# Twenty-four transposes of the identity on TensorE ahead of the first projections

## The reference, cut to what matters

```python
# q, k, v: (2, 8, 768, 64), proj: (64, 6)
q_bits = (q @ proj > 0);  k_bits = (k @ proj > 0)
bucket = sum(bits * 2 ** arange(6))                  # for q and for k
scores = 0.125 * q @ k.T, and -1e9 where the buckets of q and k differ
attn   = exp(scores - max) / (sum + 1e-9)
x = (attn @ v), heads side by side                   # (2, 768, 512)
u = x + real(fft(fft(x, axis=1), axis=2))
x2 = u + relu(layernorm(u) @ w_ch1) @ w_ch2
out = (sigmoid(causal_conv5(x2)) * (x2 @ w_val)) @ w_out
```

## Time and profile before

| | |
|---|---|
| median of 3 runs | 647.86 us (647.46 to 648.29) |
| the profiled execution, its own time | 647.66 us |
| its span, first to last instruction | 646.0 us |
| TensorE busy | 618.5 us, 96% of the span |
| VectorE / ScalarE / GpSimd busy | 353.4 / 316.9 / 245.6 us |
| mean granted TensorE clock recorded | 0.997 |

### The profile page before, as it was taken

How to read it: one execution, slowest core, us unless ns; L and a number is a source line. 1 busy time by engine, 2 the same in 40 slices (tenths; PEclk the granted TensorE clock), 3 DMA queues, 4 the chain that set the end, 5 groups by cost and what they waited for, 6 DMA issues and landing times.

```text
span 646.0 us, 11034 instructions
## 1 busy us (share of the span) xinstructions
PE 618.5 (96%) x3730; PEld 502.5 (78%) x3730; DVE 353.4 (55%) x587; ACT 316.9 (49%) x608; POOL 245.6 (38%) x199
## 2 busy tenths in 40 slices
PE   2999999999999999887999999999999999999998
PEld 1767777767767766886888888888888888888786
DVE  2888888888888885986211111115533333439820
ACT  2777777777787763465222222225332333354242
POOL 6533443334334342844322333325544444303140
PEclk9999999999999999999999999999999999999999
DMA  5662323323332000100222111431322212000202
GB/s 130 201 142 64 86 62 85 85 74 103 91 85 61 14 13 1 49 2 2 66 65 63 53 49 62 166 95 33 97 56 59 55 59 65 16 2 1 82 17 97
DMA packets 34265, 42.12 MB, mean 65 GB/s; under 512 B 3520, under 2 KB 22208, under 8 KB 34240
## 3 DMA queue, kind: packets, MB, share of 16 engines
q1 hardware_dynamic: 32512, 37.77, 20.4%
q0 software_dynamic: 1728, 4.02, 2.5%
HBM read 38.63 MB, written 3.15 MB: 65 GB/s over the span
## 4 chain that ended last, share of the span: by engine, by line
PE 86%; DVE 7%; issue 2%; POOL 2%; ACT 2%; DMA 1%; SPq 0%; ACTq 0%; DVEq 0%; POOLq 0%
PE banks L1487 21%; PE banks L1475 20%; PE banks L1285 12%; PE banks L1302 10%; PE banks L1349 9%; PE banks L1582 4%; PE banks L1241 2%; PE banks L1566 2%; PE banks L1422 2%; DVE x_then_u_then_gate L1160 1%; PE banks L1325 1%; PE banks L1247 1%; PE banks L1357 1%; POOL row_sums_and_differences L526 1%; PE banks L1396 1%
## 5 line engine op out<-in xcount | busy, mean ns | idle before, releaser
L1147 DVE SCALAR_TENSOR_TENSOR h_lo<-banks,h_hi 128x512 fp32r<-128x512 f32 x64 | 35.3, 557 | 181.3 <-ACT h_hi L809 181.3
L954 DVE TENSOR_REDUCE row_min<-banks 128x1 f32<-128x768 f32 x96 | 91.8, 956 | 33.0 <-PE banks L1285 32.5
L663 ACT ACTIVATE prob<-banks,row_min 128x768 f32<-128x768 f32 x96 | 87.0, 906 | 35.7 <-DVE row_min L954 35.6
L1475 PE MATMUL banks<-unT_hi,w_hi 128*128 128x512 f32 (+1 forms) x256 | 86.5, 338 | 0.2 <-DVE h_lo L1147 0.2
L1475 PE MATMUL banks<-unT_hi,w_lo 128*128 128x512 f32 (+1 forms) x256 | 86.2, 337 | 0.0
L1475 PE MATMUL banks<-unT_lo,w_hi 128*128 128x512 f32 (+1 forms) x256 | 86.2, 337 | 0.0
L1349 PE MATMUL banks<-ident,prob 128*128 128x128 f32 x576 | 79.3, 273 | 2.4 <-ACT probT L342 1.3
L549 POOL TENSOR_TENSOR w_lo<-w_stage,w_hi 128x512 fp32r<-128x512 f32 x32 | 45.3, 1416 | 80.9 <-ACT w_hi L726 80.9
L1349 PEld LDWEIGHTS banks<-ident,prob 128*128 128x128 f32 x576 | 68.4, 140 | 7.7 <-issue 2.4
L554 POOL TENSOR_TENSOR w_lo<-w_stage,w_hi 128x512 fp32r<-128x512 f32 x32 | 42.2, 1318 | 74.9 <-ACT w_hi L731 74.9
L1302 PE MATMUL banks<-probT,v_in 128*64 128x384 f32 x384 | 69.0, 494 | 0.7 <-DVE probT L342 0.7
(11 more groups left out here) (147 smaller groups left out, 1188.2 us busy)
## 6 DMA issues: line engine op xcount, KB each, us to landing
w_stage<-in_moe_w_ch SPq DMA_DIRECT2D x64, 256.0 KB, 2.8
q_raw<-in_q SPq DMA_DIRECT2D x32, 192.0 KB, 3.2
k_raw<-in_k SPq DMA_DIRECT2D x32, 192.0 KB, 3.6
v_in<-in_v SPq DMA_DIRECT2D x16, 192.0 KB, 2.8
out<-y_out SPq DMA_DIRECT2D x12, 256.0 KB, 2.0
seq_tables_sb<-in_dft POOLq DMA_DIRECT2D x6, 386.0 KB, 3.6
wvo_stage<-in_moe_w_val SPq DMA_DIRECT2D x1, 1024.0 KB, 5.8
wvo_stage<-in_moe_w_out SPq DMA_DIRECT2D x1, 1024.0 KB, 8.9
```

The lines of the kernel that those rows point to most:

```text
L663: act.activation(prob[s % 2][:, :, :], s_tile(s), ACT.Exp, bias=row_min[:, s:s + 1], scale=-1.0, accum_out=row_sum[:, s:s + 1]).then_inc(e ...
L954: dve.tensor_reduce(row_min[:, s:s + 1], s_tile(s), AX.XY, ALU.min).then_inc(min_ready, 1)
L1147: dve.scalar_tensor_tensor(out=h_lo[:, slot, at:at + size], in0=h_bank[c], scalar=0.0, in1=h_hi[:, slot, at:at + size].bitcast(F32), op0=A ...
L1475: op = pe.matmul(h_bank[c], w_[:, slot, kb, :], x_[:, kb, at:at + size], start=(kb == 0 and m == 0), stop=(kb == KB - 1 and m == 2))
```

## The change

Behind the wait for the identity and before the wait for `w_ready`, TensorE transposes the identity 24 times into the same 128 columns of bank 7. Nobody reads the result, no semaphore is raised, and nothing is removed or moved.

```diff
@@ -383,6 +383,8 @@
         LAG = 3
+
+        WARM = 24
@@ -1366,6 +1368,8 @@
             pe.wait_ge(consts_ready, 7)
 
+            for n in range(WARM):
+                pe.transpose(PS[:, 7, 0:P], ident[:, :], ident[:, :])
             pe.wait_ge(w_ready, 2)
             pe.wait_ge(codes_loaded, 16)
```

## The result

| | kernel before | changed kernel |
|---|---|---|
| median | 647.68 us (20 runs, 646.79 to 648.44) | 646.86 us (20 runs, 645.13 to 647.84) |
| ratio | | 0.9984, 95% interval 0.9978 to 0.9990 |
| profiled execution | 647.66 us, span 646.0 us | 646.16 us, span 644.5 us |
| mean recorded clock of it | 0.997 | 0.992 |

The kernel became 0.8 us faster, 0.16%, where 1.0 us was forecast.

The account below looks back on a forecast made before the run. TensorE, busy 96% of the span, was taken as the bound, at a low unrecorded clock until about 20.3 us. Free transposes and a faster prologue gave 647.66 - 0.95 = 646.7 us, range 644.6 to 648.1 us.

Parts of the forecast that it names:

- The cost: At the start, 24 transposes at 0.215 us each end inside the wait for `proj` and `w_k`; taken as 0.
- The rise: During or just behind the starting transposes, TensorE's clock goes to the high level, between 6.6 and 9.2 us.
- the 0.68 us of L1241: Prologue's eight L1241 matmuls, 1.54 us on the chain, take about 0.85 us at the high clock; 0.68 us saved.
- the 0.28 us of L1247: Prologue's first L1247 shrinks from 0.70 to 0.42 us at the high clock; 0.28 us saved.
- The fall: Between the transposes and the first scores TensorE is about 30% busy, so the clock falls about when the scores start.
- the comparison of three stretches: Busy shares ahead of a possible fall: 62% near 280 us held, 47% before 303.7 us fell, about 30% to come.
- the 62% stretch: From 280.30 to 284.90 us, TensorE busy 2.87 of 4.60 us, thinnest found at the high level without a fall.
- a long low stretch: From the first scores, clock low 5.9 us as before, only 0.95 us earlier: 646.7 us, likeliest case, chance 0.38.
- The short rival: From the first scores, clock low only 3.4 us, as at 303.7 us: 1.9 us saved, 645.8 us, chance 0.21.
- the row minimum of slot 2: VectorE's step that started at 20.40 us before; its new start was said to give the whole gain.
- No fall: Clock stays high through the first scores: 0.95 + 0.64 + 1.2 = 2.8 us saved, 644.8 us, chance 0.23.
- The low stretch near 303 us: Late in the kernel, said to move the end up to about 1.2 us either way, unrelated to the transposes.

Follow-up runs that it names:

- c3: The changed kernel with nothing altered, profiled once more (third look): 646.88 us, one run.
- c2: The changed kernel with nothing altered, profiled once more (second look): 647.01 us, one run.
- e7: 48 transposes at the start instead of the changed kernel's 24: 648.38 us, ratio 1.0004 to the kernel before.
- e4: The changed kernel plus 7, 7 and 8 transposes in the layer norm gaps near 300 us: 645.97 us, ratio 0.9978 to the kernel before.
- e1: The changed kernel plus 18 transposes in the gap ahead of the first scores: 644.76 us, ratio 0.9956 to the kernel before.
- e6: The changed kernel with 12 plain float32 matmuls of the identity in place of the 24 transposes: 646.66 us, ratio 0.9983 to the kernel before.
- c1: The changed kernel with nothing altered, profiled once more (first look): 646.57 us, one run.
- e5: The changed kernel plus 5 and 18 transposes before the first scores, 12 near 280 us, and 7, 7, 8 near 300 us: 644.05 us, ratio 0.9942.
- e8: The kernel before plus only late transposes, 12 near 280 us and 7, 7, 8 near 300 us: 646.78 us, ratio 0.9984.
- e2: The kernel before plus only 10 transposes in the gap ahead of the first scores, none at the start: 646.04 us, ratio 0.9975.

## Why the prediction was right

**The cost.** Taken at 0 with 0.2 to 0.4 us to spare, it was 0 with 0.4 to 1.9 us to spare (idle time ahead of L1243 in c3 and c2). L1243 starts at 8.94 instead of 8.83 us because `w_k` came later, 8.88 instead of 8.73 us, behind a load of `proj` that took 3.97 instead of 3.86 us. That all write the same columns did not matter: they followed each other at 0.21 us and less, not 0.40. Where they do outlast the cover, as the 48 of e7, the real work comes later by the excess, 2.3 us.

**The rise.** Forecast between 6.6 and 9.2 us, it came at 6.4 us in the profile, near 8.8 in e7, and in c3 (5.38 us for 24) not before the last transpose, yet L1243 was fast in every profile with 24. So the 0.68 us of L1241 and the 0.28 us of L1247 were nearly got: 1.54 to 0.90 us and 0.70 to 0.46 us, 0.88 us together. With L1243 starting 0.11 us later the first scores came 0.78 us earlier than before, at 13.66 and not at 13.49 us. Transposes alone raised the clock, as the earlier trace rows had shown once. The rule of the Trainium skill, page "TensorE: Matmul & The Clock Gate", section "Part 4: PE-mode transpose", that they do not count as busy, does not hold here: the clock rose while TensorE had done nothing but transposes, and 24 transposes and 12 matmuls of the same length acted alike.

**The fall.** The step on which the most hung was the comparison of three stretches: 62% busy, held; 47%, fell; about 30% to come. The coming one was 26% (1.47 of 5.60 us) in the profile, and the clock fell in all five profiles. With the gap filled it stayed. So the fall was rightly forecast.

The comparison behind it is weaker than it looked. The fall of e4 came behind 5.60 us that were 70% busy and that of c3 behind 5.60 us that were 65% busy (3.63 us, 6.40 to 12.00), both thicker than the 62% stretch that had held. And that 62% stretch, with its gap of 1.7 us, did not always hold either: of the eleven profiles in which it is unfilled, the clock fell within 1.7 us of the gap's end in four (e1, e4, e6, c1, at 282.6 to 284.0 us). A busy share read off one profile does not settle whether the clock falls, and that the three stretches of the comparison came out in order was in part luck.

The longest single gap ahead of the first scores was 2.50 us. The Trainium skill, same page, section "HAM oscillation — how this bites in real kernels", ties a fall to idle gaps longer than this one; three falls, this one, that of e4, and the one near 300 us behind gaps of 1.14 us at most, came without such a gap. The trace of before also held a second fall, which the prediction did not count: at 645.0 us, 2.1 us behind the last matmul, where TensorE has no work left.

**What the fall leaves.** Forecast 0.95 us with a long low stretch and 1.9 us with a short one. Measured at 248 us: 0.92, 0.82 and 0.42 with a long one, 1.50 and 1.36 with a short one. The long one was the likeliest case and its gain is that of the median. It was not the case of the profiled execution, and the median is one of a mix: two profiles of five had the short stretch, and the twenty runs of the changed kernel lie between 2.5 us below and 0.2 us above the median of before, late low stretches included. The long stretch was also longer than forecast (6.8 us, not 5.9) and began 1 to 3 us before the first scores, not with them. The short rival was sized 0.4 to 0.5 us too high: I took the row minimum of slot 2 as the end of the gain. It started 1.8 us earlier in the profile, at 17.66 + 0.96 = 18.6 us instead of 20.40, but slot 3's scores then waited 0.55 us for ScalarE and came 1.45 us earlier. So that moment does not give the whole gain, as the prediction said it would; slot 3's scores do.

**No fall.** Forecast 2.8 us, of which 1.2 us, and not TensorE's own 1.9, for the part in which the exponential leads. e1 measured 2.70 us at 247 us. This sum was made for the rival and holds for the kernel with its gap filled.

**What I treated as outside.** The low stretch near 303 us was called worth up to 1.2 us either way and left out of the sum. That was fair for this change and missed how much it carries of the run-to-run spread. These are medians of runs sorted by their mean recorded clock, those of before from e1's comparison and those of the changed kernel from the result. In that mean 3.4 us at the low level are worth 1.7 / 646 = 0.0026:

| recorded clock | low stretches of 3.4 us | before (26 runs) | changed (20 runs) |
|---|---|---|---|
| 0.999 to 1.000 | none, or less than one | 646.82 us, 7 runs | |
| 0.997 | one | 647.71 us, 15 runs | 645.13 us, 1 run |
| 0.994, 0.995 | two | 648.45 us, 4 runs | 645.84 us, 6 runs |
| 0.992 | three | | 646.87 us, 9 runs |
| 0.989 | four | | 647.62 us, 4 runs |

Each such stretch goes with 0.7 to 1.0 us here. In the 28 runs of before that e5 to e8 were compared with, the steps are 0.8 us (646.99 to 647.80) and 0.45 us (to 648.25, four runs). A changed kernel's record holds one or two more at the start, since the old low start has no record and the new one has. That is why its recorded clock is lower although it is faster. Not settled is what decides in an execution whether a low stretch is short or long; it differs between executions of one program, and so does the moment of the first rise.

## What to carry to other kernels

Judge TensorE's clock in the first microseconds by the duration of an instruction that also occurs later, since the granted clock may have no record there. Work that raises the clock is worth what the chain ahead of the next thin stretch is worth; if TensorE is mostly idle behind it, the clock falls again, and ten transposes in the gap before the dense part (e2) were worth twice the 24 at the very start. Fill the stretches in which TensorE waits on the others with work that ends before the wait does, and stop there: in e7 what exceeded the wait, 2.3 us, delayed the real work by as much and cost 1.5 us of the median. Do not trust one profile to say which thin stretch is safe: the same one held the clock in seven executions and lost it in four.

## What was unexpected of the hardware

The clock rose 3.2 us after the start of the transposes in one execution and 5.6 us after it in another (e7), in work that had no break. All recorded low stretches that ended within the kernel were 3.4 us or 6.8 us long, in the eleven profiles that had one. In e4 the clock fell while TensorE was at work, behind 5.60 us that were 70% busy. And 34 transposes in idle time near 280 and 300 us took away 0.9 us of the median that no reading of the chain had shown, since a mean clock of 0.997 looks like full speed.
